# Two expert mixtures after chunked attention: the last tile's h is turned inside the product ahead, scatters go ahead of weight pieces at the turn, and the row past the end is dropped

## What is computed

```python
def _moe_ref(x, w_gate, w_output_gate, w1, w2):      # the first mixture; N, D, E, F = 2304, 512, 8, 1024
    logits = x @ w_gate
    e_idx = np.argmax(logits, axis=1)                # one expert per row
    ...
        h = np.maximum(x[mask] @ w1[e], 0.0)         # 512 -> 1024
        ye = h @ w2[e]                               # 1024 -> 512
        out[mask] = gate_w[mask, None] * eom[mask, e, None] * ye

def reference(...):
    attn_out = _attn_ref(**attn_kwargs)              # softmax attention within chunks of 64 rows
    ...
    x = _moe_ref(x=x, **moe_kwargs)
    return _moe2_ref(x=x, **moe2_kwargs)             # second mixture: same shapes, no output gate, a capacity
```

## Time and profile before

| what | value |
|---|---|
| median of 3 runs (lowest, highest) | 706.04 us (705.34, 706.71) |
| the profiled execution, its own time | 706.62 us |
| its span, first to last record | 704.9 us |
| PE busy | 605.6 us, 86% of the span |
| DVE, POOL, ACT busy | 448.7, 406.4, 185.6 us |
| attention and first routing | to about 127 us |
| mixture 0, its last scatter issued | 396.66 us |
| second routing, to mixture 1's first product | 402.35 to 422.36 us |
| mixture 1's last scatter issued | 695.48 us |

### The profile page before, as it was taken

The page is one execution under the profiler, slowest core; times in us unless marked ns, Lnnn a source line. Parts: engine busy times, 40 slices in busy tenths (PEclk is TensorE's granted clock), DMA queues, the critical chain, the costliest instruction groups (busy, mean ns, idle before and its releaser), DMA issues.

```text
span 704.9 us, 14919 instructions
## 1 busy us (share of the span) xinstructions
PE 605.6 (86%) x4106; PEld 492.3 (70%) x4107; DVE 448.7 (64%) x1037; ACT 185.6 (26%) x241; POOL 406.4 (58%) x276
## 2 busy tenths in 40 slices
PE   4887873899999999999996139999999999999573
PEld 3766652688888888888884037888888888887462
DVE  3887757469879999889997574354543545433340
ACT  2678742022240222423321200022023200244110
POOL 1146313394797649799987210663667671779760
PEclk9999985899999999999998658999999999999796
DMA  9899860487465326566666101523434541346600
GB/s 210 215 286 282 238 214 15 166 315 265 153 224 189 120 106 216 168 202 226 199 203 207 27 17 30 166 96 105 156 128 166 174 163 46 132 160 210 221 23 16
DMA packets 79308, 113.75 MB, mean 161 GB/s; under 512 B 27737, under 2 KB 46169, under 8 KB 79152
## 3 DMA queue, kind: packets, MB, share of 16 engines
q1 hardware_dynamic: 67616, 86.00, 39.8%
q0 software_dynamic: 8000, 25.17, 10.5%
q10 hardware_dynamic: 3664, 2.20, 1.0%
HBM read 94.57 MB, written 20.00 MB: 163 GB/s over the span
## 4 chain that ended last, share of the span: by engine, by line
PE 72%; DVE 9%; issue 6%; DMA 5%; ACT 3%; POOL 2%; POOLq 1%; ACTq 1%; DVEq 0%; SPq 0%
PE b L1043 20%; PE b L1045 19%; PE b L1044 19%; PE b L1065 4%; PE b L1038 2%; POOL wl L438 2%; PE b L965 2%; DMA ring<-in_moe_w 2%; PE b L943 2%; PE b L953 1%; ACT wh L619 1%; DMA x<-y,sidx 1%; DMA out<-y,sidx 1%; DVE kT L684 1%; DMA cap_i<-in_capacity 1%
## 5 line engine op out<-in xcount | busy, mean ns | idle before, releaser
L438 POOL TENSOR_TENSOR wl<-ring,wh (+1 forms) x128 | 302.8, 2393 | 31.5 <-ACT wh L619 26.8
L619 ACT CAST wh<-ring 128x1024 f32 (+1 forms) x112 | 113.0, 1048 | 398.2 <-PE b L1045 314.4
L1043 PE MATMUL b<-wh,hTh 128*128 x320 | 132.5, 414 | 11.7 <-DVE hTl L857 11.7
L1043 PE MATMUL b<-wh,xTh 128*128 x320 | 131.4, 411 | 5.5 <-DVE xTl L844 3.7
L1044 PE MATMUL b<-wh,hTl 128*128 x320 | 128.7, 402 | 0.0
L1045 PE MATMUL b<-wl,hTh 128*128 x320 | 128.6, 402 | 0.0
L1045 PE MATMUL b<-wl,xTh 128*128 x320 | 127.9, 400 | 0.0
L1044 PE MATMUL b<-wh,xTl 128*128 x320 | 127.6, 399 | 0.0
L880 DVE SCALAR_TENSOR_TENSOR unread<-b,gates,wg_rows 128x512 f32<-128x512 f32 x160 | 110.1, 745 | 1.2 <-PE b L1045 1.2
L829 DVE TENSOR_SCALAR h<-b 128x512 f32<-128x512 f32 x80 | 55.5, 696 | 55.6 <-PE b L1045 54.1
L866 DVE CAST sidx<-b 128x1 int32 (+1 forms) x40 | 6.6, 164 | 129.2 <-PE b L1045 67.3
(11 more groups left out here) (147 smaller groups left out, 640.2 us busy)
## 6 DMA issues: line engine op xcount, KB each, us to landing
ring<-in_moe_w SPq DMA_DIRECT2D x128, 512.0 KB, 3.3
vin<-in_v SPq DMA_DIRECT2D x72, 64.0 KB, 4.3
x<-xrow POOLq DMA_DIRECT2D x18, 256.0 KB, 5.6
out<-zeros SPq DMA_DIRECT2D x18, 256.0 KB, 3.5
qin<-in_q SPq DMA_DIRECT2D x6, 512.0 KB, 6.9
kin<-in_k SPq DMA_DIRECT2D x6, 512.0 KB, 6.0
wg_rows<-in_moe_w_gate ACTq DMA_DIRECT2D x1, 2048.0 KB, 7.1
qin<-in_q SPq DMA_DIRECT2D x2, 384.0 KB, 5.7
```

The lines of the kernel that those rows point to most:

```text
L438: nc.gpsimd.tensor_tensor(low, src, high.bitcast(F32), ALU.subtract).then_inc(wl_here, 1)
L619: nc.scalar.copy(dst, ring[:, i % RING]).then_inc(wh_here, 1)
L1043: nc.tensor.matmul(dst, high, weights(wh, *wt), start=start, stop=False)
```

## The change

It takes step 18 (`total - 2`) out of the loops of the PE and DVE and writes it out as `nearly`. In it the PE turns no rows of a tile 20, and turns `h` of tile 19 between the two halves of tile 18's second product. DVE splits no rows and copies no index for tiles past the end; behind relu and `scaled` (in mixture 0 `scaled(17)`) it splits the turned `h` of tile 19, and only then does `next_logits(18)` (mixture 0) and `scaled(18)`. The last step is then the second product of tile 19 on the PE, and its logits and `scaled` on DVE. On POOL the gather of tile 20 is gone. In mixture 0 step 18 scatters tile 16 ahead of its pieces 68 to 71, and the last step scatters tiles 17, 18 and 19, and then takes its pieces 72 to 75. In mixture 1 the order on POOL is the old one.

```diff
@@ POOL @@
-                def step(g, ahead=True):
+                def step(g, ahead=True, first=False):
                     lo, middle, hi = due(m, g)
+                    if first:
+                        scatter(g - behind)
                     split(lo, middle)
-                    if reached(g, behind):
+                    if reached(g, behind) and not first:
                         scatter(g - behind)
...
-                with pool.Fori((3, 1)[m], total - 2) as g:
+                with pool.Fori((3, 1)[m], total - 3) as g:
                     step(g)
-                step(total - 2, ahead=False)
-                step(total - 1, ahead=False)
-                if m == 0:
+                step(total - 3, ahead=False)
+                step(total - 2, ahead=False, first=(m == 0))
+                if m == 1:
+                    step(total - 1, ahead=False)
+                    scatter(total - 1)
+                else:
+                    lo, _, hi = due(0, total - 1)
+                    scatter(total - 3)
                     scatter(total - 2)
-                scatter(total - 1)
+                    scatter(total - 1)
+                    split(lo, hi)
@@ DVE @@
+                    if nearly:
+                        for half in range(2):
+                            hidden_high(g + 1, half)
+                            hidden_low(g + 1, half)
-                    if m == 0 and tail:
+                    if m == 0 and (nearly or tail):
                         next_logits(g, range(E))
-                    if m == 1 or tail:
+                    if m == 1 or nearly or tail:
                         scaled(g)
@@ PE @@
+                    if tail:
+                        second_product(g, *last_one)
+                        return
...
+                    last_one.extend(following)
+                    second_product(g, *this, halves=(0,))
+                    hidden_T(g + 1, 0)
+                    hidden_T(g + 1, 1)
+                    second_product(g, *this, halves=(1,))
```

More of the change, by code:

```diff
@@ L313, in expert_steps @@
             step(0)
-            with eng.Fori(1, total - 1) as g:
+            with eng.Fori(1, total - 2) as g:
                 step(g)
+            step(total - 2, nearly=True)
             step(total - 1, tail=True)
@@ L882, in next_logits, with step @@
                             op0=ALU.mult, op1=ALU.mult, accum_out=next_lg[:, e:e + 1]).then_inc(next_lg_here, 1)
-                def step(g, head=False, tail=False):
+                def step(g, head=False, nearly=False, tail=False):
                     if head:
@@ L892, in step @@
                         return
[L893 to L896, removed]
                     if not tail:
+                        hidden_high(g, 0)
+                        hidden_high(g, 1)
+                        hidden_low(g, 0)
+                        hidden_low(g, 1)
                         relu(g + 1, 0)
-                    if m == 0 and reached(g, 1):
-                        next_logits(g - 1, range(0, E // 2))
-                    if not tail:
+                        if m == 0 and reached(g, 1):
+                            next_logits(g - 1, range(0, E // 2))
                         relu(g + 1, 1)
+                    if not tail and not nearly:
                         next_rows(g + 3)
                         x_split(g + 2)
-                    if m == 0 and reached(g, 1):
+                    if m == 0 and reached(g, 1) and not tail:
                         next_logits(g - 1, range(E // 2, E))
@@ L1066, in hidden_T, with second_product @@
                     last.then_inc((hT0_done, hT1_done)[half][m], 1)
-                def second_product(g, first, before):
+                def second_product(g, first, before, halves=(0, 1)):
                     dst = result_bank(pe, g)
[L1070 to L1073, removed]
+                    if 0 in halves:
+                        pe.wait_ge(wl_here, before + PX)
+                        if reached(g, 1):
+                            pe.wait_ge(y_here[m], g)
+                    for half in halves:
                         pe.wait_ge((hT0_here, hT1_here)[half][m], g + 1)
@@ L1077, in second_product, with step @@
                                            start=(c == 0), stop=(c == FC - 1))
-                    last.then_inc(y_done[m], 1)
-                def step(g, head=False, tail=False):
+                    if 1 in halves:
+                        last.then_inc(y_done[m], 1)
+                last_one = []
+                def step(g, head=False, nearly=False, tail=False):
                     if head:
@@ L1087, in step @@
                         return
+                    if tail:
+                        second_product(g, *last_one)
+                        return
                     this = expert_of(g)
-                    if not tail:
-                        following = expert_of(g + 1)
+                    following = expert_of(g + 1)
                     hidden_T(g, 0)
                     hidden_T(g, 1)
-                    if not tail:
-                        first_product(g + 1, 0, *following)
-                        first_product(g + 1, 1, *following)
+                    first_product(g + 1, 0, *following)
+                    first_product(g + 1, 1, *following)
+                    if not nearly:
                         rows_T(g + 2)
-                    second_product(g, *this)
+                        second_product(g, *this)
+                        return
+                    last_one.extend(following)
[3 more added lines that the diff above has]
+                    second_product(g, *this, halves=(1,))
                 expert_steps(pe, m, step)
```

## The result

The change makes the kernel slower: 709.10 us (704.95 to 710.16) against 705.38 (703.52 to 707.61), 12 runs each on one chip, a ratio of 1.0046 with an interval of 1.0032 to 1.0061, that is 3.2 us (2.3 to 4.3). The changed kernel timed once more, beside the kernel before, gave 708.74 against 706.44, 1.0036 (1.0014 to 1.0057), 2.5 us (1.0 to 4.0). Its two large terms of opposite sign are both there; each came out some tenths less good than forecast.

A forecast was written before the change was run, and what follows sets the result against it. The PE is busy 86% of the span, so an edit leaving the loops alone pays only at the mixtures' two ends. Routing 5.3 later less 4.0 gained is +1.3 us: 707.4 on the 706.04 median, range 705.9 to 709.8.

The forecast's parts named there:

- Sum 1: Mixture 0 up to scatter 19: the scatter goes at 390.85, 5.8 us earlier than before.
- the PE doesn't hold this up: End of mixture 0: the PE finishes its last product at 382.0 or 383.9, against tile 19's logits at 383.6.
- Sum 2: From scatter 19 to the second routing: pieces delay casts and the logits load, so routing starts at 407.6, 5.3 us later.
- the wait for a cast's end: Rival on ACT before the second routing: logits load waits for the last cast's end, 1.0 more, 708.3; chance 0.07.
- a load that passes the casts: Rival on ACT: logits load passes waiting casts, routing 5.8 earlier, sum -9.8 us, 696.3; passing casts' chance 0.09.
- all but the first of them: Rival variant on ACT: only the first of four casts holds the logits load, routing 1.7 earlier, sum -5.7, 700.3.
- The block behind the routing: From the second routing to mixture 1's end, only the loop's last turn is edited; all shifts with the routing, 5.3 later.
- Sum 3: End of mixture 1: last product starts 2.45 us earlier and runs 1.5 shorter, gain 4.0, bounds 2.4 and 4.2.
- written-out steps cost fetches: Rival for the written-out last steps: fetches, or a longer landing, cost 0 to 1.5 us either way; chance 0.09.
- I take it that the clock stays up: Mixture 1's last product: after a 2.1 us gap it takes 5.7 us in place of 7.2, 1.5 more gained.
- the clock's rival: Clock falls in the short gaps: mixture 1 loses 1.5 us, mixture 0 some 0.3, sum +3.1, 709.2; chance 0.13.

The follow-up runs named there:

- the change again: The changed kernel, unedited, timed once more beside the kernel before: 708.74 us against 706.44, ratio 1.0036 (1.0014 to 1.0057).
- mixture 0 alone: The change's edits kept only in mixture 0, mixture 1 as in the kernel before: ratio 1.0090 (1.0058 to 1.0123) to the kernel before.
- POOL's order of before: The changed kernel with POOL's old order (pieces, then scatter) in both last steps of mixture 0: 703.40 us, ratio 0.9966 to the kernel before.
- ACT's order changed: The changed kernel with ACT's wait for the scatters, logits load and exponentials ahead of the casts of pieces 76 to 79: 701.83 us, ratio 0.9945.
- Mixture 1 alone: The change's edits kept only in mixture 1, mixture 0 as in the kernel before: ratio 0.9938 (0.9914 to 0.9963) to the kernel before.
- pieces behind the routing: The changed kernel with ACT's logits load and exponentials ahead of its last four casts, and POOL's four pieces behind mixture 1's third gather: 696.77 us, 0.9866.
- three pieces and one: The changed kernel with three of POOL's last four pieces between scatters 17 and 18, the fourth between 18 and 19: 698.41 us, ratio 0.9875.

## Why the prediction was right, and where its sizes were off

- **Sum 1, scatter 19 5.8 earlier: right, but for "the PE doesn't hold this up".** Net of A it went at 391.4, 391.0 and 390.5 in the change, the change again and mixture 0 alone; forecast 390.85. In the first of them the slow product held DVE up for 0.61; in the other two the product ran at full clock and there was no such wait. The prediction itself had the PE out at 383.9 with slow stretches in it, against 383.6. The pivotal step was that scatter 16 goes first; POOL's order of before shows that the rest is worth little without it.
- **Sum 2, routing 5.3 later: right in its links, 0.3 short.** The maximum came 5.8, 5.5 and 5.7 later. From scatter 19 to the maximum the change took 16.76 and 16.77, where the forecast has 16.75, so there what was short is scatter 19; mixture 0 alone took 17.50, with a last piece's load of 4.06 where the change had 3.45 and 3.27. That the casts hold up the load of the logits is shown by moving them (ACT's order changed), and that it needs only the last cast's start by the 0.08 between them. With them fall two rivals, the wait for a cast's end, and a load that passes the casts, or all but the first of them. The Trainium skill ("Perfetto Trace Analysis", "DVE / Act Engine Instruction") has the sequencer ready for the next instruction once one is in the wait queue; these rows disagree, as rows 9 and 10 had.
- **The block behind the routing.** I shifted it as it stood. It came 5.5, 6.2 and 6.0 later at mixture 1's third tile (relu at 448.1 before), some 0.6 more than 5.3; half is Sum 2's 0.3, the rest lies in the routing and the first gathers, where single executions differ as much. In the change again, part of it is the clock: the halves of mixture 1's first relu stand 3.14 apart (432.29 and 435.43; 2.80 before), with 0.85 granted over the 2 us behind the first, where before had 1.00. What the remainder is is not settled.
- **Sum 3, mixture 1 gains 4.0: right alone, 3.6 in the change.** Mixture 1 alone gave 4.0 from C to D. In all seven profiled executions of kernels with both mixtures' edits on DVE a stall of 0.47 stands ahead of the last `y`, worth 0.4; in the four of kernels with one of them or none there is no such row. The rival "written-out steps cost fetches" had this kind of price. That it is a fetch is my reading: the row only says that no semaphore held it. One thing beside it is in the DMA view of after, 697.5 to 698.5, queue, packets, MB, share:

```profile
q14 instruction: 1, 0.01, 2.4%
```

  One packet of the queue that the profile calls instruction goes by 0.6 to 0.9 us behind the start of the last `y` in each of the seven, and in none of the other kernels at this place. So the two go together. But the packet comes behind the stall, so it isn't what DVE waited for, and the view doesn't name its engine; the stall's cause stays open.
- **The clock.** I took it that it stays up after 2.1 us of idle. In the eight profiled executions with mixture 1's edit it did in six, and in two (POOL's order of before, pieces behind the routing) 0.67 was granted and the product took 1.5 longer. In mixture 0 seven executions have such a short gap; four stayed up, and in three (the change, ACT's order changed, three pieces and one) 0.57 to 0.61 was granted over the product's first 4 us. There it costs less, since DVE is busy beside it: its wait for the product was 0.61, 0.62 and 0.45. So the rival happens in some executions. In mixture 1 it costs about 2/8 of 1.5, 0.4 us on the mean over them, an estimate from eight executions of seven kernels; in mixture 0 its cost is in the 5.8, 5.5 and 5.7 already. What tells the executions apart is open.

With those sizes the sum is 5.9 - 3.6 + 0.4 = +2.7 in place of 5.3 - 4.0 = +1.3, and the times say 3.2 and 2.5. What was mis-sized is thus "I take it that the clock stays up", the shifted block, and the stall that was put at nothing, each a few tenths; none is wrong in sign, but all fell to the same side. That the time still lies in the range is owed in part to its width: it had been drawn to hold the clock's rival at 709.2, and the 709.1 measured is near that by chance as far as the traces show: in both traces of the change the last product of mixture 1, where that rival has its 1.5, ran at full clock.

## What to carry to other kernels

Before moving work behind something, follow what it releases: the pieces were idle time's work on POOL, but their slots fed loads, the loads fed casts, and the casts stood ahead of the one load that the next stage needs. A gain that waits behind a queue like that is lost whole, here a scatter 5.7 us earlier (mean of three) became a routing 5.6 later, while another place for the same pieces (in POOL's waits, or behind the routing with ACT's load first) makes the kernel 0.9 to 1.3% faster instead. And time two traces from a mark ahead of the edit, else their difference is mostly not the edit's.

## What the runs showed of the hardware beyond that

- DVE's comparison with both operands in SBUF took 3.69 us instead of 0.40 while POOL ran its subtractions, which also read two operands in SBUF; it began at 400.73, inside the third of four pieces of 2.31, and ended at 404.4, behind the fourth. DVE's own subtraction `hTl`, which reads one operand from PSUM, keeps its pace beside them. Before, DVE's timeline, two of them while POOL's pieces ran from 373.55 to 382.84:

```profile
380.14 1.28 DVE L857 TENSOR_TENSOR hTl<-b,hTh 128x512 fp32r<-128x512 f32 x2
```

  The Trainium skill ("SBUF — State Buffer", section "SBUF: two separate sides") has a port pair shared by the two engines, which whoever starts first holds for its whole instruction. The rows agree on who waits; but they show that DVE didn't get in between the third and fourth pieces, so here, in the one case traced, a row of back-to-back instructions on POOL held DVE for more than one.
- After 1.94 to 2.10 us of idle ahead of a last product the granted clock of its first 4 us was 1.00 in ten executions and 0.57 to 0.67 in five. The length of the gap doesn't tell them apart: behind 1.94 us it fell three times and stayed up at others, behind 2.10 it stayed up once.
